# Turning attention outputs with VectorE and DRAM transfers instead of TensorE, in an attention and channel-mix kernel

## The reference, cut to what matters

```python
# attention: q, k, v are (4, 8, 1152, 64)
q_pool = q.reshape(B, H, S // 2, 2, D).mean(axis=3)          # 576 queries a head
scores = scale * np.matmul(q_pool, k.transpose(0, 1, 3, 2))
scores = scores - np.max(scores, axis=-1, keepdims=True)
attn = np.exp(scores)
attn = attn / (np.sum(attn, axis=-1, keepdims=True) + 1e-09)
attn_out = np.matmul(attn, v)
x = attn_out.transpose(0, 2, 1, 3).reshape(B, S // 2, H * D)  # (4, 576, 512)
# mix
mu, var = mean(x), mean((x - mu) ** 2)                        # over the last axis
xn = (x - mu) / np.sqrt(var + 1e-06) * g_ln
out = x + np.maximum(xn @ w_ch1, 0.0) @ w_ch2                 # 512 -> 2048 -> 512
```

## Time and profile before

| | |
|---|---|
| time, median of 3 runs | 792.25 us (792.03 to 792.56) |
| profiled execution, its own time | 791.6 us |
| its span in the profile | 789.8 us |
| TensorE matmuls busy | 781.0 us, 99% of the span |
| VectorE busy | 643.1 us, 81% |
| ScalarE busy | 424.8 us, 54% |
| GpSimd busy | 436.4 us, 55% |
| TensorE clock granted | 1.0 of full speed |
| DMA | 84.80 MB in 80433 packets |

### The profile page before, as it was taken

The page is one execution under the profiler, slowest core; times in us unless marked ns, Lnnn a source line. Parts: engine busy times, 40 slices in busy tenths (PEclk is TensorE's granted clock), DMA queues, the critical chain, the costliest instruction groups (busy, mean ns, idle before and its releaser), DMA issues.

```text
span 789.8 us, 17026 instructions
## 1 busy us (share of the span) xinstructions
PE 781.0 (99%) x6398; PEld 654.4 (83%) x6398; DVE 643.1 (81%) x1010; ACT 424.8 (54%) x946; POOL 436.4 (55%) x338
## 2 busy tenths in 40 slices
PE   8999999999999999999999999999999999999998
PEld 6777778777777777778779899999999998999897
DVE  6987988878888989988799779898778898766655
ACT  4676566765566755667853446543345444233431
POOL 3899988888888889988887024411211431131100
PEclk9999999999999999999999999999999999999999
DMA  8566533665345653435331354213356212512212
GB/s 190 138 150 150 126 83 91 150 150 131 83 106 131 149 143 84 98 93 138 87 79 54 96 158 120 68 54 123 108 128 168 74 56 67 173 55 68 59 37 81
DMA packets 80433, 84.80 MB, mean 107 GB/s; under 512 B 47200, under 2 KB 62048, under 8 KB 76768
## 3 DMA queue, kind: packets, MB, share of 16 engines
q1 hardware_dynamic: 80192, 83.65, 41.1%
q10 hardware_dynamic: 160, 0.07, 0.0%
HBM read 74.25 MB, written 9.44 MB: 106 GB/s over the span
## 4 chain that ended last, share of the span: by engine, by line
PE 92%; DVE 5%; issue 1%; ACT 1%; POOL 0%; DVEq 0%; ACTq 0%; POOLq 0%
PE banks L1395 25%; PE banks L1384 20%; PE banks L803 16%; PE banks L792 14%; PE banks L736 5%; PE banks L790 4%; DVE pm L1120 2%; PE banks L1362 2%; PE banks L819 2%; DVE acc_end L1066 1%; PE banks L830 1%; PE banks L744 1%; PE banks L864 1%; PE banks L769 0%; DVE q_sums L611 0%
## 5 line engine op out<-in xcount | busy, mean ns | idle before, releaser
L639 POOL TENSOR_TENSOR acc<-acc,pT 128x576 f32<-128x576 f32 x160 | 237.3, 1483 | 23.2 <-ACT pT L995 0.4
L1395 PE MATMUL banks<-w2f,hT 128*128 128x512 f32 x858 | 211.6, 391 | 0.0
L995 ACT ACTIVATE pT<-banks 128x576 f32<-128x576 f32 x288 | 171.6, 659 | 36.5 <-PE banks L790 31.6
L1120 DVE TENSOR_REDUCE pm<-banks 128x2 f32<-128x1024 f32 x128 | 153.5, 1222 | 39.8 <-PE banks L736 38.0
L1395 PEld LDWEIGHTS banks<-w2f,hT 128*128 128x128 f32 x858 | 159.8, 188 | 28.3
L792 PE MATMUL banks<-qT,kT 64*128 64x288 f32 x1728 | 162.5, 298 | 1.9 <-DVE pm L1120 1.2
L792 PEld LDWEIGHTS banks<-qT,kT 64*128 64x128 f32 x1728 | 133.9, 184 | 17.0 <-DVE pm L1120 6.7
L803 PE MATMUL banks<-pT,vn 128*64 128x288 f32 x1152 | 145.9, 407 | 0.0
L1473 ACT ACTIVATE hT<-mid 128x384 fp32r<-128x384 f32 x88 | 46.2, 525 | 173.4 <-DVE mid L1540 172.8
L439 POOL TENSOR_TENSOR w_sums<-w_stage 128x256 f32<-128x256 f32 x22 | 17.4, 792 | 219.8 <-DMA w_stage<-in_moe_w_ch_dram 208.0
L1540 DVE TENSOR_TENSOR mid<-banks,mid 128x384 f32<-128x384 f32 x154 | 85.5, 555 | 54.1 <-PE banks L1384 48.8
(11 more groups left out here) (129 smaller groups left out, 960.5 us busy)
## 6 DMA issues: line engine op xcount, KB each, us to landing
q_in_rows<-in_q_dram SPq DMA_DIRECT2D x56, 284.0 KB, 6.7
k_in_rows<-in_k_dram SPq DMA_DIRECT2D x56, 284.0 KB, 5.2
w_stage<-in_moe_w_ch_dram SPq DMA_DIRECT2D x24, 512.0 KB, 4.6
w_stage<-in_moe_w_ch_dram SPq DMA_DIRECT2D x48, 256.0 KB, 2.7
vn<-in_v_dram SPq DMA_DIRECT2D x16, 576.0 KB, 5.2
tokens<-xn SPq DMA_DIRECT2D x18, 256.0 KB, 2.8
token_sums<-tokens SPq DMA_DIRECT2D x72, 64.0 KB, 2.6
out_dram<-x SPq DMA_DIRECT2D x15, 256.0 KB, 3.2
```

What stands on the lines that cost most here:

```text
L639: nc.gpsimd.tensor_tensor(total, pT[:, h % 2, 0] if kt == 1 else total, pT[:, h % 2, kt], ALU.add).then_inc(chained, 1)
L995: nc.scalar.activation(pT[:, h % 2, kt], pair_banks("S", n)[:, :, 0:HW], ACT.Exp, scale=SCALE).then_inc(exp_done, 1)
L1120: nc.vector.tensor_reduce(pm[:, at // GROUPS, :, at % GROUPS], src, AX.X, ALU.max).then_inc(max_taken, 1)
L1395: last = nc.tensor.matmul(banks[:, k % 2 * (CT // 2) + kk], hT[:, k, a, tokens], w2f[:, (2 * u + k // 2) % 4, b], start=p == 0 and k < 2 a ...
```

## The change

For pairs 0 to 12 (`SENT = PAIRS - 3` = 13 of them) the outputs go another way. VectorE turns each half out of PSUM into `oT` in 32 x 32 blocks (`turn_values`, steps `P` for the second half of the pair before, first in a round, and `p` for this pair's first half). SP sends a pair's `oT` to a DRAM tensor in four transfers whose pieces are 32 numbers long (`send_outputs`) and fetches it into `x` in two (`fetch_outputs`). ScalarE multiplies it by `inv` in place, ten instructions of 64 columns a pair, behind step `L` (`scale_fetched`). Pairs 13 to 15 stay with ScalarE's copy, TensorE and VectorE. `O` leaves `PAIR_STEPS`, `L` moves from banks 0 and 1 to 6 and 7. The queries' sum `s` moves from VectorE to GpSimd, behind its last add of a round. `LATE` reaches to round 13. Variance plus 1e-6 and the scaled mean are made by GpSimd, here and in the mix.

```diff
+    SENT = PAIRS - 3
+    outputs = nc.dram_tensor("outputs", (SENT, NQ, 2 * DH), f32, kind="Internal").ap()
...
-                  "S@6 M@4 S@0 O@6 E@3 L@0 PV@2 KQ@4 KA@6 SH@3 Z@1 PV@0")
+                  "S@6 M@4 S@0 E@3 L@6 PV@2 KQ@4 KA@6 SH@3 Z@1 PV@0")
...
-    VECTOR_STEPS = "m m m m m a m m m m e l c o Q K a q k s"
-    VECTOR_LATE = "m m m m m m m m m e l c o Q K a q k a s"
-    LATE = range(2, PAIRS - 7)
+    VECTOR_STEPS = "P m m m m m a m m m m e l c Q K p a q k"
+    VECTOR_LATE = "P m m m m m m m m m e l c Q K p a q k a"
+    LATE = range(2, PAIRS - 2)
-    VECTOR_0 = "l e m m c m e m m m l m m m m m c a Q K a q k s"
+    VECTOR_0 = "l e m m c m e m m m l m m m m m c a Q K p a q k"
...
         def inverse_deviation(n):
+            nc.gpsimd.wait_ge(moments_ready, CT * (n + 1))
+            nc.gpsimd.tensor_tensor(var_eps[:], moments[:, :, 1], eps[:], ALU.add).then_inc(var_ready, 1)
...
-                    eng.wait_ge(pv_copied, m + 1)
+                    eng.wait_ge(*((out_turned, m + 1) if m < 2 * SENT else (pv_copied, m - 2 * SENT + 1)))
...
+            def send_outputs(j):
+                sp.wait_ge(out_turned, 2 * (j + 1))
+                for r in range(128 // BLOCK):
+                    rows = slice(r * BLOCK, (r + 1) * BLOCK)
+                    sp.dma_start(outputs[j, :, rows].rearrange("(b i) e -> i b e", i=BLOCK),
+                                 oT[rows, j % 2, 0:NQ].rearrange("i (b e) -> i b e", e=BLOCK)).then_inc(outputs_sent[j % 2], 16)
+            def fetch_outputs(j):
+                sp.wait_ge(outputs_sent[j % 2], 64 * (j // 2 + 1))
+                wait(sp, outputs_in[j % 2], 32 * (j // 2))
+                whole, (_, rows), end_tile = query_slices(j)
+                tile, cols = whole[0][1], slice(j % BP * 128, (j % BP + 1) * 128)
+                sp.dma_start(x[:, tile:tile + FULL, cols],
+                             outputs[j, 0:FULL * 128].rearrange("(t p) c -> p t c", t=FULL)).then_inc(outputs_in[j % 2], 16)
+                sp.dma_start(x[rows, end_tile, cols], outputs[j, FULL * 128:NQ]).then_inc(outputs_in[j % 2], 16)
...
             for j in range(3, PAIRS):
                 if j > 3:
                     load_values(j - 3)
+                    send_outputs(j - 4)
                 sp.wait_ge(q_summed, j)
                 load_queries(sp, j)
+                if j > 3:
+                    fetch_outputs(j - 4)
                 load_keys(j)
             load_values(PAIRS - 3)
+            send_outputs(PAIRS - 4)
             send_tokens(sp, 0, 0)
             send_tokens(sp, 0, 1)
+            fetch_outputs(PAIRS - 4)
...
                 add_rest(2 * j + 1)
+                if j + 3 < PAIRS:
+                    next_queries(j + 3)
...
+            def scale_fetched(j):
+                act.wait_ge(sums_inv, j + 1)
+                act.wait_ge(outputs_in[j % 2], 32 * (j // 2 + 1))
+                whole, (_, rows), end_tile = query_slices(j)
+                for s in range(2):
+                    cols = slice(j % BP * 128 + s * DH, j % BP * 128 + (s + 1) * DH)
+                    for t in range(FULL):
+                        at = x[:, whole[t][1], cols]
+                        nc.scalar.mul(at, at, inv[:, t, s:s + 1])
+                    at = x[rows, end_tile, cols]
+                    last = nc.scalar.mul(at, at, inv[rows, FULL, s:s + 1])
+                last.then_inc(x_written, 1)
...
                     scalar_step(kind, n)
+                    if kind == "L" and n > 2:
+                        scale_fetched(n - 3)
...
+            def turn_values(h):
+                j, c = h // 2, h % 2
+                wait(dve, outputs_sent[j % 2], 64 * (j // 2))
+                dve.wait_ge(pv_done, h + 1)
+                nc.vector.transpose(oT[:, j % 2, c * HW:(c + 1) * HW].rearrange("p (b e) -> p b e", e=BLOCK),
+                                    pair_banks("PV", h)[:, 0, 0:HW].rearrange("p (b i) -> p b i", i=BLOCK)).then_inc(out_turned, 1)
```

More of the change, by code:

```diff
@@ L175, in pooled_attention_channel_mix @@
         rstd = sb("rstd", [128, CT])
-        minus_mean = sb("minus_mean", [128, CT])
+        half_mean = sb("half_mean", [128, CT])
+        half_shift = sb("half_shift", [128, CT])
+        eps = sb("eps", [128, CT])
         shift = sb("shift", [128, CT])
@@ L244, in pooled_attention_channel_mix @@
         o_turned, x_written = sem("o_turned"), sem("x_written")
+        out_turned = sem("out_turned")
+        outputs_sent, outputs_in = [sem(f"outputs_sent{i}") for i in range(2)], [sem(f"outputs_in{i}") for i in range(2)]
         sums_made, w1_hi, w1_lo, w2_hi, w2_lo = (sem("sums_made"), sem("w1_hi"), sem("w1_lo"), sem("w2_hi"),
@@ L620, in attention_gpsimd @@
             nc.gpsimd.memset(minus_half[:], -0.5).then_inc(half_made, 1)
-            pool.wait_ge(half_made, 1)
+            nc.gpsimd.memset(eps[:], 1e-6).then_inc(half_made, 1)
+            pool.wait_ge(half_made, 2)
             pool.wait_ge(zeros_made, 1)
@@ L670, in attention_gpsimd @@
                 add_rest(2 * j + 1)
+                if j + 3 < PAIRS:
+                    next_queries(j + 3)
                 if j == PAIRS - 5:
                     inverse_deviation(0)
+                    nc.gpsimd.tensor_tensor(half_mean[:], moments[:, :, 0], minus_half[:], ALU.mult).then_inc(mean_ready, 1)
                     pool.wait_ge(mean_ready, 1)
                     pool.wait_ge(rstd_ready, 1)
-                    nc.gpsimd.tensor_tensor(shift[:], minus_mean[:], rstd[:], ALU.mult).then_inc(mean_ready, 1)
+                    nc.gpsimd.tensor_tensor(half_shift[:], half_mean[:], rstd[:], ALU.mult).then_inc(mean_ready, 1)
+                    pool.wait_ge(mean_ready, 2)
+                    nc.gpsimd.tensor_tensor(shift[:], half_shift[:], half_shift[:], ALU.add).then_inc(mean_ready, 1)
         def turn_first_keys(pe, j):
@@ L824, in turn_outputs @@
         def turn_outputs(pe, j):
-            pe.wait_ge(pv_copied, 2 * (j + 1))
+            pe.wait_ge(pv_copied, 2 * (j - SENT + 1))
             whole, (end, _), _ = query_slices(j)
@@ L903, in scale_outputs @@
             g = j % BP
-            nc.vector.wait_ge(o_turned, j + 1)
+            nc.vector.wait_ge(o_turned, j - SENT + 1)
             nc.vector.wait_ge(sums_inv, j + 1)
@@ L1020, in scalar_step @@
                     shifts(n)
-                elif kind == "PV":
+                elif kind == "PV" and n >= 2 * SENT:
                     copy_values(n)
@@ L1188, in attention_vector @@
                         joined += 1
-                    elif op == "o" and j > 1:
-                        scale_outputs(j - 2)
+                    elif op == "P" and 0 < j <= SENT:
+                        turn_values(2 * j - 1)
+                    elif op == "p" and j < SENT:
+                        turn_values(2 * j)
                     elif op == "Q" and j + TURNED < PAIRS:
@@ L1201, in attention_vector @@
                         added += 1
[L1202 to L1205, removed]
                 if j in (PAIRS - 7, PAIRS - 6, PAIRS - 5):
@@ L1406, in down @@
                 if u == 0 and k == 0:
-                    pe.wait_ge(pv_copied, HALVES)
+                    pe.wait_ge(pv_copied, HALVES - 2 * SENT)
                     pe.wait_ge(z_copied, PAIRS)
```

11 lines of the change are left out of this document (3 added, 8 removed).

## The result

The changed kernel takes 787.04 us (median of 4 runs, 786.88 to 787.48) beside 792.18 us before (792.03 to 792.56, 4 runs): ratio 0.9935, 95% interval 0.9922 to 0.9948, 5.1 us faster. The profiled execution took 787.15 us, its span is 785.4. The forecast was 783.5 with a range of 781.9 to 787.4, so the time lies in the range, near its upper end. It does not lie in the forecast's own range of 782.0 to 785.5, and 3.5 us of the forecast's 8.7 are missing. First, in which stage.

What follows compares the result with a forecast made beforehand. TensorE, 92% of the chain, was taken as the bound. From 791.6 us, 8.4 + 0.5 + 0.6 gained and 0.25 + 0.25 + 0.3 lost gave 782.9, or 783.5 as median; range 781.9 to 787.4, the forecast's own 782.0 to 785.5.

Steps and rivals of the forecast that it cites:

- a VectorE that is late in every round: Rival, 12 in 100: each round's first maximum comes 0.3 us late on VectorE, giving 787.1 us.
- TensorE's turns: Five turns of outputs a round removed from TensorE in rounds 2 to 14: 0.70 us a round, 8.4 for 12 rounds.
- L's bank: Rest scores moved from bank 0 to bank 6: round 1 gains 0.5 us, the other rounds lose nothing.
- `s` off VectorE: The queries' sum leaves VectorE, so round 2's late first maximum goes: 0.6 us gained.
- `P`: VectorE's turn of the second half's values: 0.45 us, making the first maximum 0 to 0.1 us later a round.
- LATE and statistics: Late order up to round 13 gains 1.17 us; statistics in rounds 9 to 11 lose 1.4: net loss 0.25.
- ScalarE: Ten multiplications a pair, 2.7 us, hidden by idle time except in round 14.
- Round 14: ScalarE's fullest round: the 0.70 us from removed turns is spent and 0.25 more lost, as round 15's first exponential starts late.
- GpSimd: With the queries' sum, 23.5 us of work fits a 23.7 us round; 0.3 us charged at the end, before the last row sums.
- The rival in which it paces the rounds: Rival, 12 in 100: GpSimd's work, from 24.1 us a round, paces the rounds: 788.7 us, or 786 in half of them.
- Transfers: Sends and fetches of outputs through DRAM: 1.8 us of 16 engines a round for the sends, cost 0.
- The slow rival, a late fetch: Rival, 4 in 100: ScalarE waits for the fetch before scaling and holds up TensorE's inputs: 809 us.

Runs made afterwards that it cites:

- after_l0: The changed kernel with step L back on banks 0 and 1, without O in front of it: 794.86 us, ratio 1.0032 to the kernel before.
- after_s_dve: The changed kernel with the queries' sum of pairs 3 and on back on VectorE at the end of its order: 789.97 us.
- after_late9: The changed kernel with the late order taken out of all rounds from 9 on, leaving it in rounds 2 to 8: 787.00 us.
- before_pad64: The kernel before with one unused tile of 64 B per partition ahead of the tile shift, nothing else: 795.07 us, ratio 1.0029.
- after_place0: The changed kernel with seven small tiles and `one` packed into one tile, so later tiles lie where they lay before the change: 784.44 us.

## Why the prediction was nearly right, and where it was not

The mechanism was right; the sum was 3.5 us too good in the medians, and 4.3 (8.7 against 4.4) between the two profiled executions: 2.9 in the mix, 0.6 before the first values, 0.7 in the attention (7.96 against 8.7). The step that failed is one that the sum did not have: the mix, taken as untouched. That the range held is in part luck. Its upper part was there for a VectorE that is late in every round (787.1), and this did not happen; a loss that no rival named gave nearly the same time. Step by step:

* **TensorE's turns**, 0.70 a round: measured 24.39 - 23.75 = 0.64. The turns had hidden 0.07 of what now stands between the last scores and the values (0.85 against 0.78). Over 12 rounds 0.7 less than charged.
* **L's bank**, +0.5 in round 1: the stretch from round 0's values to round 1's went from 23.41 to 22.95, 0.46, and `after_l0` shows what the move is worth in the other rounds, which is all that the turns gave.
* **`s` off VectorE**, +0.6: round 2's stretch gained 1.22, 0.58 beyond the ordinary 0.64. `after_s_dve` confirms it and adds the statistics' rounds, to 2.9 in all.
* **`P`**: 0.48 us each against 0.45, the first maximum 0.53 behind the values against 0.55 before. Charge of 0 to 0.1: 0.
* **LATE and statistics**: charged 0.3 + 0.3 + 0.8 = 1.4; 0.27 + 0.66 + 0.27 = 1.20. Right in sum, with the peak in round 10 and not in 11. `after_late9` shows that the extension itself earns nothing: the 0.15 that an `a` among the maxima cost before (24.54 against 24.39) is gone in the changed kernel in the ordinary order too (23.74 and 23.76). Why was not tried.
* **ScalarE**: 2.87 us against 2.7, hidden by idle time as forecast. In round 15 the first exponential starts at 381.24, 2.2 behind the values' end at 379.02 (forecast 2.4).
* **Round 14**: the two stretches behind round 13's values were 46.33 and are 47.03: 0.70 lost where 0.25 was charged. The missing part starts earlier than I looked. Round 14 has the ordinary order, with an `a` among the maxima. It took 1.79 us there, where it took 1.52 in the kernel before, and TensorE stood 0.47 for the maximum behind it, against 0.19 before. After, on VectorE and TensorE, and then the same two rows before:

```profile
362.50 1.79 DVE L1121 TENSOR_TENSOR acc_end<-pT 128x576 f32<-128x576 f32 x1
364.21 3.57 DVE L1175 TENSOR_REDUCE pm<-banks 128x2 f32<-128x1024 f32 x3
```

```profile
365.48 0.67 PE L828 MATMUL banks<-qT,kT 64*128 64x288 f32 x6 [0.47 <-DVE pm L1175]
```

```profile
370.56 1.52 DVE L1066 TENSOR_TENSOR acc_end<-pT 128x576 f32<-128x576 f32 x1
373.27 0.67 PE L792 MATMUL banks<-qT,kT 64*128 64x288 f32 x6 [0.19 <-DVE pm L1120]
```

* **GpSimd**: the 23.5 us a round were right. The queries' sum is its last work of a round, and with a lag to work off it comes every 23.2 to 23.5 us, as here in rounds 7 and 8 (timeline of GpSimd):

```profile
213.47 1.42 POOL L641 TENSOR_TENSOR q_sums<-q_in_rows 128x576 f32<-128x576 f32 x1
236.87 1.43 POOL L641 TENSOR_TENSOR q_sums<-q_in_rows 128x576 f32<-128x576 f32 x1
```

The 22.32 of the stretches is less, because it leaves out the short gaps between adds, as the 20.62 of the earlier trace rows does. The sum started 15.5 us behind the first half's values in round 1, 11.5 in round 10, and 12.4 in round 12, behind the small operations: the lag shrinks slowly, as forecast. The last add ended at 406.11, 1.9 ahead of the row sums at 407.97, so the 0.3 for the tail was not paid. The rival in which it paces the rounds is out, by 0.25 us a round. Longer is `a`, 1.345 us on average against 1.111. That is not the queries' sum alone: in `after_l0`, which has it too, `a` takes 1.180, and in `after_s_dve`, which has it on VectorE, 1.290. When `a` meets the adds seems to matter more, which is not shown; why it would meet them worse in the shorter rounds was not tried.
* **Transfers**: no cost seen, and none when doubled. SP stood 2.1 us in all for sends to land, in 4 of the 13 fetches, and TensorE's rounds show nothing of it (23.7 to 23.8). The slow rival, a late fetch, is out: ScalarE's waits at the scaling are all for `inv`.
* **The mix**: 2.92 us, of which `before_pad64` and `after_place0` put 2.5 to 2.9 down to three small tiles. Without it the changed kernel takes 784.44, 0.9 from the forecast.

What stays open is the mechanism of the placement: which tile behind the pad `xf` has to suit, and why down matmuls, whose own operands `hT` and `w2f` keep their distance in all these kernels, change their pace with the tile that the products ahead of them read.

## What to carry to other kernels

A change to one stage also moves the tiles of every later stage: compare the untouched stages' length first, and if it differs at the same count and clock, pad or pack small tiles until the old addresses are back. Work removed from the bounding engine is often cover for a wait; look for the round that lacks it already, as round 1 did, and move the wait in the same edit. A sum with two SBUF inputs beside a busy GpSimd should be costed at its longest case, because it is the longest one that makes the next maximum late.

## What the runs showed of the hardware

* Moving the tiles behind the pad (`w1f`, `hT`, `w2f`, `xf_more`) by 64 B against `xf` slowed the mix's matmuls by 1.0% to 1.5% at the same clock (9 in 2.05 to 2.08 us, 12 in 2.08 to 2.10) and cost 2.7 to 2.9 us of 381; moving all five together cost nothing; another 64 B gave 2.04 and 2.12. Groups of products that read `xf_more` had the slow pace in every kernel. No sign of it in attention's rounds.
* Stores of 128 B pieces to DRAM cost 14.9 ns of one DMA engine each, fetched ones 12.7; a send of 72 KB landed in 3.8 us (median).
* VectorE's block transpose of 288 columns out of PSUM takes 0.48 us; a ScalarE multiplication of 64 columns in SBUF 0.34 alone, and four in a row take 1.06.
